# Query and key tiles laid out by head in natural order, with the head dimension split into halves instead of even and odd columns

## The reference

```python
# q, k, v: (4, 8, 768, 64); n_sink = 4, window = 128
scores = scale * np.matmul(q, k.transpose(0, 1, 3, 2))
keep = is_sink | in_window                     # last 128 positions and the first 4
a = softmax(np.where(keep, scores, -1e9))
x = np.matmul(a, v)                            # -> (3072, 512), heads side by side
a = x @ w1; b = x @ w2
x = (a * b @ w3) @ w_out
e_idx = argmax(x @ w_gate + modality_bias[modality_id])
out = gate_w * (np.maximum(x @ w1[e], 0) @ w2[e])   # e = e_idx, 8 experts, D 512, F 1024
```

## Time and profile before

| what | value |
|---|---|
| median of 3 runs | 923.55 us (922.85 to 924.24) |
| profiled execution, its own time | 922.85 us |
| its span, first to last instruction | 921.2 us |
| PE busy, PEld busy | 899.2 us, 836.5 us |
| DVE, ACT, POOL busy | 598.4, 383.2, 178.6 us |
| granted TensorE clock, mean | 0.996 |
| bytes moved, mean rate | 83.32 MB, 90 GB/s |

### The profile page before, as it was taken

How to read it: one execution, slowest core, us unless ns; L and a number is a source line. 1 busy time by engine, 2 the same in 40 slices (tenths; PEclk the granted TensorE clock), 3 DMA queues, 4 the chain that set the end, 5 groups by cost and what they waited for, 6 DMA issues and landing times.

```text
span 921.2 us, 21191 instructions
## 1 busy us (share of the span) xinstructions
PE 899.2 (98%) x7602; PEld 836.5 (91%) x7602; DVE 598.4 (65%) x1453; ACT 383.2 (42%) x933; POOL 178.6 (19%) x289
## 2 busy tenths in 40 slices
PE   7999999999999999999999999999999999999995
PEld 6778899999999999999999999999999999999994
DVE  6776675685675685675685672277566666666655
ACT  3557343342342443333333332251555455555553
POOL 2451112232221241231322221011100000000000
PEclk9999999999999999999999999999999999999998
DMA  7635523122132222222221212144711116111111
GB/s 229 196 116 180 199 75 94 50 77 86 50 90 79 69 70 70 70 74 74 70 82 59 80 37 82 37 159 161 253 46 46 46 45 227 43 44 42 41 41 33
DMA packets 80180, 83.32 MB, mean 90 GB/s; under 512 B 46303, under 2 KB 56543, under 8 KB 80096
## 3 DMA queue, kind: packets, MB, share of 16 engines
q1 hardware_dynamic: 75568, 68.54, 24.3%
q0 software_dynamic: 4240, 13.66, 3.9%
q10 hardware_dynamic: 288, 0.00, 0.0%
HBM read 56.70 MB, written 25.74 MB: 89 GB/s over the span
## 4 chain that ended last, share of the span: by engine, by line
PE 84%; DVE 9%; issue 3%; ACT 2%; DMA 1%; DVEq 0%; ACTq 0%; POOL 0%; SPq 0%; POOLq 0%
PE acc_b L329 5%; PE acc_b L331 5%; PE acc_b L330 5%; PE acc_a L329 5%; PE acc_a L330 4%; PE acc_a L331 4%; PE attn L979 4%; PE misc L323 4%; PE misc L324 4%; PE misc L325 4%; PE s_even L942 3%; PE acc_a L323 3%; PE attn L325 2%; PE attn L324 2%; PE acc_b L323 2%
## 5 line engine op out<-in xcount | busy, mean ns | idle before, releaser
L810 POOL TENSOR_TENSOR probs<-scores,row_inv 128x256 f32<-128x256 f32 x96 | 67.3, 723 | 306.5 <-DVE row_inv L1857 306.5
L1349 ACT ACTIVATE ew<-raw_e 128x1024 fp32r (+1 forms) x100 | 101.2, 1050 | 13.6 <-issue 13.6
L329 PE MATMUL acc_b<-xT_w,w 128*128 128x384 f32 x256 | 88.6, 346 | 2.1 <-DVE ab L1901 2.1
L329 PE MATMUL acc_a<-xT_w,w 128*128 128x384 f32 x256 | 90.2, 352 | 0.0
L330 PE MATMUL acc_b<-xT_w,w 128*128 128x384 f32 x256 | 86.5, 338 | 0.0
L331 PE MATMUL acc_b<-xT_w,w 128*128 128x384 f32 x256 | 86.5, 338 | 0.0
L330 PE MATMUL acc_a<-xT_w,w 128*128 128x384 f32 x256 | 86.5, 338 | 0.0
L331 PE MATMUL acc_a<-xT_w,w 128*128 128x384 f32 x256 | 86.4, 338 | 0.0
L1375 ACT ACTIVATE scores<-scores,neg_max 128x136 f32<-128x136 f32 x192 | 75.7, 398 | 11.2 <-DVE neg_max L1847 11.1
L1991 DVE TENSOR_TENSOR ew<-raw_e,ew 128x1024 fp32r<-128x1024 f32 x52 | 60.4, 1219 | 28.6 <-ACT ew L1349 28.6
L1349 ACT ACTIVATE uT_w<-ab 128x384 fp32r<-128x384 f32 x64 | 33.5, 523 | 105.1 <-DVE ab L1901 105.1
(11 more groups left out here) (357 smaller groups left out, 2894.0 us busy)
## 6 DMA issues: line engine op xcount, KB each, us to landing
raw_e<-in_moe_w SPq DMA_DIRECT2D x24, 512.0 KB, 6.5
raw<-in_moe_w SPq DMA_DIRECT2D x16, 512.0 KB, 6.4
x_in<-routed SPq DMA_DIRECT2D x29, 257.0 KB, 2.9
v_nat<-in_v SPq DMA_DIRECT2D x24, 256.0 KB, 2.9
x_mid<-x_out SPq DMA_DIRECT2D x24, 256.0 KB, 2.0
x_in<-x_mid SPq DMA_DIRECT2D x24, 256.0 KB, 2.7
q_nat<-in_q SPq DMA_DIRECT2D x80, 64.0 KB, 2.3
k_nat<-in_k SPq DMA_DIRECT2D x80, 64.0 KB, 1.9
```

What stands on the lines that cost most here:

```text
L329: pe.matmul(o, w_hi, x_hi, start=start, stop=False, skip_group_check=True)
L810: pool.tensor_tensor(probs[:, at, side * HALF:(side + 1) * HALF], scores[:, at, side, SINKS:], row_inv[:, at].unsqueeze(2).broadcast_to([P ...
L1349: return act.activation(o, i, ACT.Copy)
```

## The change

The order of the columns becomes the natural one on both sides. Lot `e` is now the first or the second 32 values of a head. Quarter `part` holds heads 0 and 2, 1 and 3, 4 and 6, 5 and 7. So `scores` and `probs` hold the heads in natural order, `place_of` is gone, and the views of `of_head` are plain.

In `turn_qk` VectorE reads neighbouring columns instead of every second one; what it writes is unchanged, in place and in step. For tiles 4 to 23 the loads keep their number, size and run length (four DMAs for q, four for k), only from other heads.

For tiles 0 to 3 a plain load no longer gives an arrangement that TensorE can transpose in one piece, so each head is loaded by its own DMA, which cuts the 64 values of a token in two runs of 32 values (128 bytes): 8 DMAs for q and 8 for k, 32 KB each, instead of one and one of 256 KB in runs of 256 bytes. TensorE's transposes then read neighbouring columns. The counts that TensorE and VectorE wait for on `qk_in` follow.

```diff
-        def place_of(h):
-            return h % 2 + h // 2 % 2 * 4 + h // 4 * 2
+        def heads_of(part):
+            first = 4 * (part // 2) + part % 2
+            return slice(first, first + 3, 2)
...
-            return x[b, part:H:4, i * P:(i + 1) * P, :].rearrange("a (j f) d -> j a (f d)", f=4)
+            return x[b, heads_of(part), i * P:(i + 1) * P, :].rearrange("a (j f) d -> j a (f d)", f=4)
+
+        def head_in(home, h):
+            g, a, odd = h // 4, h // 2 % 2, h % 2
+            return home[:, :].rearrange("p (a e r n) -> p a e r n", a=2, e=2, r=4)[:, a, :, 2 * g + odd, :]
+
+        def head_of(x, b, i, h):
+            return x[b, h, i * P:(i + 1) * P, :].rearrange("s (e n) -> s e n", e=2)
...
                 if t.by_pe:
-                    sp.dma_start(heads(q_nat[:, :]), rows(q, t.b, t.i)).then_inc(qk_in, 16)
-                    sp.dma_start(heads(k_nat[:, :]), rows(k, t.b, t.i)).then_inc(qk_in, 16)
+                    for x, home in ((q, q_nat), (k, k_nat)):
+                        for h in range(H):
+                            sp.dma_start(head_in(home, h), head_of(x, t.b, t.i, h)).then_inc(qk_in, 16)
...
-                pe.wait_ge(qk_in, 32 * t.no + 32)
+                pe.wait_ge(qk_in, 32 * H * t.no + 32 * H)
...
-                    mm = pe.transpose(left[:, c * P:(c + 1) * P], q_nat[:, c // 2 * 256 + c % 2:(c // 2 + 1) * 256:2], ident[:, :])
+                    mm = pe.transpose(left[:, c * P:(c + 1) * P], q_nat[:, c * P:(c + 1) * P], ident[:, :])
...
-                                 k_nat[:, a * 256:(a + 1) * 256].rearrange("p (f n e) -> p e f n", f=4, e=2)).then_inc(qk_turned, 1)
+                                 k_nat[:, a * 256:(a + 1) * 256].rearrange("p (f e n) -> p e f n", f=4, e=2)).then_inc(qk_turned, 1)
...
-                                 q_nat[:, a * 256:(a + 1) * 256].rearrange("p (f n e) -> p e f n", f=4, e=2)).then_inc(qk_turned, 1)
+                                 q_nat[:, a * 256:(a + 1) * 256].rearrange("p (f e n) -> p e f n", f=4, e=2)).then_inc(qk_turned, 1)
```

More of the change, by code:

```diff
@@ L918, in attn_transposes @@
                 for c in range(PAIRS):
-                    mm = pe.transpose(right[:, c * P:(c + 1) * P], k_nat[:, c // 2 * 256 + c % 2:(c // 2 + 1) * 256:2], ident[:, :])
+                    mm = pe.transpose(right[:, c * P:(c + 1) * P], k_nat[:, c * P:(c + 1) * P], ident[:, :])
                 mm.then_inc(right_full, 1)
@@ L978, in attn_values @@
                             r = D * (h % 2)
-                            mm = pe.matmul(attn[r:r + D, c * P:(c + 1) * P], v_nat[:, slot, h * D:(h + 1) * D], pT[:, place_of(h), :],
+                            mm = pe.matmul(attn[r:r + D, c * P:(c + 1) * P], v_nat[:, slot, h * D:(h + 1) * D], pT[:, h, :],
                                            start=i == 0 and c == 0, stop=slot == i % 3, skip_group_check=True)
@@ L1769, in tables @@
                 ve.wait_ge(prep, 25)
-                ve.tensor_scalar(of_head[:, :].rearrange("p (a g o) -> p g a o", a=2, g=2),
-                                 expert_no[0:3 * SROWS, :].rearrange("p (g a o) -> p g a o", a=2, g=2),
-                                 part_f[0:3 * SROWS, 0:1], None, ALU.is_equal).then_inc(tables_ready, 1)
+                ve.tensor_scalar(of_head[:, :], expert_no[0:3 * SROWS, :], part_f[0:3 * SROWS, 0:1], None, ALU.is_equal).then_inc(tables_ready, 1)
                 ve.tensor_scalar(selector[:, :], expert_no[:, :], part_f[:, 1:2], None, ALU.is_equal).then_inc(tables_ready, 1)
@@ L1795, in turn_qk @@
             def turn_qk(t):
-                ve.wait_ge(qk_in, 32 * BY_PE + 32 * t.turns + 128)
+                ve.wait_ge(qk_in, 32 * H * BY_PE + 32 * t.turns + 128)
                 ve.wait_ge(scores_full, 4 * t.no)
```

## The result

| | before | after |
|---|---|---|
| median | 923.27 us (922.85 to 924.24) | 930.81 us (929.71 to 931.53) |
| ratio | | 1.0079 [1.0061, 1.0097] |
| profiled execution, its own time | 922.85 us | 931.01 us |
| its span | 921.2 us | 929.4 us |

The change costs 7.5 us in the medians (four runs each) and 8.2 us in the two profiled executions. The forecast was 925.1 us and the range ended at 928.5: wrong, and clearly outside.

What follows compares the result with a forecast made beforehand. TensorE was taken to bound the kernel; 922.85 us plus 1.6 us of wait at tile 0, all other terms 0, gave 924.45, and with 0.70 us up to the median 925.1 us; range 922.3 to 928.5.

Steps and rivals of the forecast that it cites:

- What bounds the kernel: TensorE, busy 98% of the span and 84% of the last chain; the place to look at is tile 0.
- The wait at tile 0: Before tile 0's transposes TensorE waits for the sixteen loads, the last landing at 18.4 us: 1.6 us, range 0 to 3.2.
- the pace of an issue: SyncE's issues of tile 0's head loads take 0.47 us each, the last starting at 16.5 us.
- The upper end: At tile 0, only four loads in at 13.0 us, the last landing at 20.0: a wait of 3.2 us.
- Little gives it back: TensorE's later waits in this stage follow its own work and shift with it, so little of tile 0's wait returns.
- What is queued behind: SyncE's list comes up to 6.4 us later per tile; w3 chunks 2 and 4 and x of tile 1 cost 0.
- the rival of a second late transfer: w3 chunk 4, issued at 44.0 us, lands 2.5 us late; with tile 0's wait 4.1 us, 927.7 us; chance 0.22.
- wrong if TensorE waits on a DMA anywhere but at tile 0: Sign that the prediction is wrong: any TensorE wait on a DMA at a place other than tile 0.
- TensorE's transposes: Weight loads from neighbouring columns take 141 ns instead of 210, but matmuls cover them: 0 to -0.1 us, taken as 0.
- VectorE's transposes: The 80 transposes of 256 columns stay at about 630 ns: taken as 0, with -1.8 us as the other end.
- a faster VectorE: Rival: reading was the slow side, -1.8 us; 923.3 us with tile 0's wait (chance 0.13), 921.7 without (0.07).
- The second stage: Sign that the prediction is wrong: the second stage changes its length by more than 1 us.

Runs made afterwards that it cites:

- e3_warm: The changed kernel with thirty transposes of the identity, results unused, on TensorE ahead of those of tile 0; 928.68 us, ratio 1.006.
- e5_write: The changed kernel with VectorE's transposes of q and k (tiles 4 to 23) writing neighbouring columns instead of every fourth; its one execution took 931.01 us.
- e2_split: The kernel before, with tiles 0 to 3 loaded by one DMA per head, in whole runs of 256 bytes; 923.75 us, ratio 1.0003.
- e8_two_heads: The kernel before, with q and k of tiles 0 to 3 each in four DMAs of two heads, runs of 256 bytes; 924.06 us, ratio 0.9999.
- e4_w2_early: The changed kernel with the four chunks of w2 issued before q and k of tile 3 instead of behind x of tile 1; 930.35 us, ratio 1.007.
- e6_tile0: The changed kernel with q and k of tile 0 alone loaded as before, in one DMA each; 925.36 us, ratio 1.0014.
- e10_four: The changed kernel with four of the eight DMAs for k of tile 0 issued by ScalarE ahead of its first conversion; 928.95 us, ratio 1.006.
- e9_pool: The changed kernel with the eight DMAs for k of tile 0 issued by GpSimd behind its constants; 926.65 us, ratio 1.0039.
- e11_only0: The changed kernel with tiles 1 to 3 loaded as before, one DMA each for q and k; tile 0 keeps sixteen; 929.19 us, ratio 1.0065.
- e7_act: The changed kernel with all eight DMAs for k of tile 0 issued by ScalarE ahead of its first conversion; 931.2 us, ratio 1.0073.

## Why the prediction was wrong, step by step

**What bounds the kernel: right.** All of the loss but some tenths is a stop of TensorE or its slow clock, and the first is at tile 0, as said.

**The wait at tile 0: right in kind, too small by 2.3 us.** The forecast's 1.6 us were how much later the transposes start. That was 3.91 us: TensorE was 0.33 us late already and lost 3.58 us there (3.35 of it marked as idle). The step that failed is the pace of an issue. The fill of the queue was met: the forecast had the first issue of k start at 13.2 us, and it started at 13.28. From there seven more steps of 0.47 us would have started the last at 16.6, the 16.5 of the forecast. It started at 18.5, as six steps took 0.65 us and one 1.27. The pace makes 1.3 us of the miss, the one step in which SyncE was held makes 0.6, and the landing, 2.2 us instead of 1.9, makes 0.3. The 0.47 came from loads of 64 KB in runs of 1 KB, the nearest row there was, but four times less cut up. The upper end, 3.2 us, had the same 0.47 in it; with 0.65 the same sums give 2.9 us and an upper end of 5.3.

**The clock: not in the sum at all.** It cost 1.6 us. The trace of before had a price for it that was not looked up. TensorE stands still for 6.0 us at the very start, and the first four transposes then take 1.09 us where four take 0.66 a little later:

```profile
5.99 1.09 PE L991 MATMUL attn<-ident,raw 128*128 128x128 f32 x4 [5.99 <-DMA raw<-in_moe_w]
...
9.71 0.66 PE L991 MATMUL s_even<-ident,raw 128*128 128x128 f32 x4 [0.17 <-DMA raw<-in_moe_w]
```

The range for the wait reached 3.2 us, and with an end so long the clock after it should have been asked about. "Little gives it back" was right: 0.06 us came back in 71 us.

**What is queued behind: partly wrong.** For `w3` chunks 2 and 4 and `x` of tile 1 the forecast of 0 held, as the waits near 23 and 46 us did not come, but by luck. Chunk 4 was issued 13.5 us later than before (44.69 against 31.23), where the forecast took 9, and landed at 48.2 us. At the 46.3 us of the forecast TensorE would have waited for it, by an estimate from these two numbers 1.9 us; it was spared by being 5.4 us late, and `e3_warm`, 3.7 us late, had this wait. Chunk 2 was issued at 20.74 instead of 18.1 and landed 3.8 us later, at 24.5, after the 23.6 us at which the forecast had TensorE want it.

And the list was followed to `x` of tile 1 and no further. `x` of tile 2 was the one that came late and cost TensorE 2.1 us, 1.25 at once and the rest right behind. A shift of the list was treated as if it moved issues only; here it moved 2.1 MB of weights next to a store that had been alone. So the rival of a second late transfer was right in kind. Its condition (a shift over 10 us, chunk 4 issued at 44.0) came true, but the late transfer that cost time was another one, and its 4.1 us in all would have been too little as well. The sign "wrong if TensorE waits on a DMA anywhere but at tile 0" came true at 97.36 us, by way of ScalarE and VectorE.

**TensorE's transposes and VectorE's transposes: right.** TensorE's weight loads from `q_nat`, 210 ns before, got shorter and it moved nothing:

```profile
L924 PEld LDWEIGHTS left<-ident,q_nat 128*128 128x128 f32 x16 | 1.8, 146 | 3.9 <-DMA k_nat<-in_k 3.8
```

VectorE's transposes stayed at 628 to 643 ns. The Trainium skill, Advanced Engine Details and Errata, Memory Cachelines (two hits on a line of 16 bytes give full speed), fits both sides of VectorE's transposes: `e5_write` shows that the writing side, with one hit on a line, is the slow one. It does not fit TensorE's weight loads, where every second column, two hits on a line, took 210 ns and neighbouring columns 146. The -1.8 us that the prediction put on a faster VectorE would have been too much: `e5_write` got about 0.5.

**The second stage: its sign of being wrong came true.** The forecast called itself wrong if this stage changed its length by more than 1 us. From the first product of group 0 to the first of group 7 it grew by 1.84 us (from 6.68 to 8.52). Of that 0.87 us are the rest of the late `x` of tile 2, by 99 us, and 0.87 us come at 561 us; in the 420 us between the two it grew by 0.10.

The 0.87 us at 561, where TensorE takes the first product of group 7, stand in the profiles of the change, of `e2_split`, `e8_two_heads` and `e4_w2_early` (0.6 to 0.7 us of it idle), in part in `e6_tile0` (0.5) and `e10_four` (0.4), and with 0.15 us or less in the others. `e2_split` and `e8_two_heads` have them in their slowest executions and are no slower in the median. The cause is open. It looks like something that comes in single executions, and the 0.6 us between the profiled difference (8.2) and that of the medians (7.5) may be part of it.

No run with the new loads in all of tiles 0 to 3 reaches the kernel before; the best is `e9_pool`, 0.4% above it.

## What to carry to other kernels

When one transfer is cut in many, work out the issues on the engine that makes them, with a duration from runs of the same length, and ask whether that engine's list has room at the point where the first consumer waits; a queue with large transfers in front makes it worse. When a list of transfers moves, follow it to its end and look at what each large one comes to stand in front of. A consumer that is late hides other late transfers: before such a wait is put at nothing, ask whether it would come back once the first one is mended. And price a stop of TensorE of 2.5 to 4.3 us at 1.4 to 1.7 times its length; stops of 1.0 to 1.8 us had no such price here.

## What the runs showed of the hardware

- An issue on SyncE took 0.43 us for 128 runs of 256 bytes, 0.47 for 256 runs of 256 bytes and 0.61 for 256 runs of 128 bytes; on GpSimd the last took 0.72 us. While 3 MB of weights were queued, the same issues took 0.65 us (128 runs) and 1.06 us (256 runs of 128 bytes) on the average of eight, and 1.24 us (256 runs of 256 bytes) on that of four.
- After stops of TensorE of 1.00, 1.15, 1.63 and 1.77 us (`e9_pool`, `e3_warm`, `e10_four`, `e5_write`) the granted clock stayed at 1.00. After 2.54, 2.86, 3.35 and 3.72 us (`e10_four`, `e5_write`, the change, `e4_w2_early`) it was 0.50 for 3.4 us, which cost 1.4 to 1.6 us on top of them. Around 3.69 and 4.28 us (`e11_only0`, `e7_act`) it was 0.50 for 6.8 us, which cost 2.6 and 2.2 us.
- A store of 256 KB landed in 2.15 us with 12.8 us or more between it and 2.1 MB of loads, in 2.40 us with 9.1 us, and in 4.3 to 5.6 us with 6.2 to 6.5 us between them.
- A transpose of 256 columns of four-byte values on VectorE took 403 to 423 ns when it wrote neighbouring columns and 628 to 643 ns when it wrote every fourth; reading every second column cost nothing. A weight load of TensorE from every second column of four-byte values took 210 ns, from neighbouring columns 146 ns.
